# Who loads the second image's queries: 24 small loads moved from ScalarE's queue to SyncE's, and one pair of transposes moved later on VectorE

## The chip, the cores and the metric

The kernel runs on one core of a Trainium2 chip. The metric is the device time of one execution in microseconds (us). An execution has five instruction streams: TensorE (PE, with its weight loads shown as PEld), VectorE (DVE), ScalarE (ACT), GpSimd (POOL) and SyncE (SP). SP, ACT and POOL also issue DMA transfers; a DMA issued by SP or ACT stands in the profile as an instruction of the queue SPq or ACTq. The streams meet only through semaphores, and each executes its own instructions in the order in which they are written.

## The reference, cut to what is computed

```python
# attention in chunks of 64 tokens; q, k, v: (8, 8, 576, 64)
scores = scale * q_c @ k_c.T                  # 64 x 64 in each chunk of each head
attn = exp(scores - rowmax); attn = attn / (rowsum + 1e-9)
x = attn @ v_c                                # put together as (8, 576, 512)
# first layer: token mixing, then channel mixing
u = x + (relu(x.T @ w_tok1) @ w_tok2).T       # 576 -> 256 -> 576 tokens
x = u + relu(u @ w_ch1) @ w_ch2               # 512 -> 1536 -> 512 channels
# second layer: a gated layer
h = relu(x @ w_in); u, v = halves of h
v_n = (v - mean(v)) / sqrt(var(v) + 1e-6)
out = (u * (w_spatial @ v_n + b_spatial)) @ w_out
```

Everything is float32. A product is made of three passes over operands split in a high and a low part, so each weight matrix needs a high copy (written by ACT) and a low remainder (computed by POOL) before TensorE uses it.

## The kernel before, in words

There are eight images (b = 0 to 7) of 576 tokens. Attention works on five token tiles of an image, t = 0 to 4: four of 128 tokens and one of 64. "Tile (1, 2)" is tile 2 of image 1.

**The blocks.** After a prologue that does the attention and the token mixing of image 0, the channel mixing runs in nine blocks j = 0 to 8 of 512 tokens. A block is a list of 24 groups, `GROUPS`, in an order written out by hand: g = 0 up 0, g = 1 up 1, g = 2 down 0, g = 3 up 2, g = 4 down 1, g = 5 up 3 and so on, so that down 3 is g = 8, up 5 is g = 9, down 4 is g = 10 and up 9 is g = 17. "up f" computes a slice of the hidden layer (L1194), "down f" adds its product to the result (L1209); each is 12 matmuls. Behind each group TensorE does small side jobs of the next image's attention. For block 0 they stand in `PLAN_0` (L67): scores SC.0 behind g = 4, transposes of the probabilities PT.0 behind g = 6, values PV.0 and SC.1 behind g = 7, PT.1 behind g = 9, PV.1 and SC.2 behind g = 10, PT.2 behind g = 12, PV.2 and SC.3 behind g = 13, PT.3 behind g = 15, PV.3 and SC.4 behind g = 16, PT.4 behind g = 18.

**A tile's way.** The keys and queries of images 1 to 7 come in as blocks of 32 x 32 (tiles `kn`, `qn`, two buffers each), 16 DMAs for the keys and 16 for the queries of a tile: quarters z = 0 to 3 times head pairs g = 0 to 3. VectorE's `turn(b, t)` (L839) waits for all 16 of each and transposes the blocks, k_t first and then q_t, each into its only buffer. Then come the scores on TensorE, `softmax_shift` on VectorE (L849), the exponentials on ACT (L691), and `softmax_norm` on VectorE (L863): a sum (L868), a small addition (L870), a reciprocal (L872) and a product (L874). Only then can TensorE do PT. PT.t also waits until VectorE has taken PV.(t-1) out of its bank (L878, tile xl). On VectorE the order is written out: behind the scores of tile t come `softmax_shift(t)`, `turn(t + 1)`, `softmax_norm(t)`, the remainder xl of PV.(t-1), and then the remainder of the next hidden slice (L881, tile hidl).

**Who issues the loads.** SP issues all of a tile's 16 key DMAs and quarter 0 of its queries (4 DMAs); ACT issues quarters 1 to 3 (12 DMAs), three behind each of four successive groups. Only of tile (1, 0) does SP issue all 32. In block 0, `QUERIES[True]` (L726) lists the group at which ACT begins for each of the `TILES` (L727): (1, 3) at g = 5, (1, 4) at g = 8, (2, 0) at g = 12, (2, 1) at g = 16, (2, 2) at g = 20, (1, 1) at g = 0, (1, 2) at g = 3. Before the first query DMA of a tile that stands second or later after tile (1, 0), both queues wait until the turn of the tile before last has been done (L475, L735); SP waits alike before the keys (L481).

**SP's order in the prologue.** SP issues the channel weights in six pairs (w_ch1 and w_ch2 slices, 512 KB each), with these loads between them: behind pair 1 the 32 loads of tile (1, 0), behind pair 2 the 16 key loads of (1, 1) and its 4 query loads, behind pair 3 the 16 key loads of (1, 2); behind the last pair the 4 query loads of (1, 2). Then it goes on with keys and queries of (1, 3), (1, 4), (2, 0), (2, 1) and (2, 2).

**Weights of the channel mixing.** ACT makes the high copies of pair f right behind the activation of hidden slice f (L708, called at L744), and POOL follows with the two remainders (L611).

Of the kernel before, what the change touches and what calls it, by code (L numbers as in the profile page):

```python
# [18 lines left out]
def jobs(b, text):  # L19
    return [(kind, b, int(t)) for kind, t in (x.split(".") for x in text.split())]  # L20


def build(nc, q, k, v, w_tok1, w_tok2, w_ch1, w_ch2, w_in, w_spatial, b_spatial, w_out, out, x2_dram):
# [22 lines left out]
    def rows(t):  # L46
        return P if t < KS else REM
# [24 lines left out]
    def behind(j, g):  # L72

        if j > B - 1:
            return []
        side = jobs(j, (REST if j > 0 else REST_0).get(g, ""))
        if j < B - 1:
            return side + jobs(j + 1, (PLAN if j > 0 else PLAN_0).get(g, ""))
        return side + jobs(0, SPATIAL.get(g, ""))

    def scores_first(side):
        return [job for job in side if job[0] == "SC"] + [job for job in side if job[0] != "SC"]
# [46 lines left out]
    with ExitStack() as ctx:  # L129
# [10 lines left out]
        def place(name, shape, dt, at):  # L140
            t = nc.alloc_sbuf_tensor_at(name, shape, dt, offset=at)
            nbytes = 4
            for n in shape[1:]:
                nbytes *= n
            return t, at + (nbytes + 31) // 32 * 32
# [21 lines left out]
        qn, at = place("qn", [P, 2, PAIRS * P], F32, zone_a)  # L167
# [109 lines left out]
        def sem(name):  # L277
            return ctx.enter_context(nc.semaphore(name))
# [4 lines left out]
        q_loaded = [sem(f"q_loaded{t}") for t in range(NT)]  # L283
# [88 lines left out]
        q_in, k_in, v_in = q, k, v  # L372

        def later(b, t):

            return (b - 1) * NT + t
# [25 lines left out]
        def blocks(buf, b, t):  # L402
            return buf[:, later(b, t) % 2, 0:PAIRS * rows(t)]

        def block_of(buf, src, b, t, z, g):

            dst = blocks(buf, b, t)[z * BLK:(z + 1) * BLK, :].rearrange("p (g j e) -> p g j e", g=PAIRS, e=BLK)
            part = src[b, 2 * g + z // 2, t * P:t * P + rows(t), z % 2 * BLK:(z % 2 + 1) * BLK]
            return dst[:, g, :, :], part.rearrange("(j r) e -> r j e", r=BLK)
# [52 lines left out]
        def _(sp):  # L462
# [4 lines left out]
            def load_blocks(buf, src, b, t, loaded, quarters=range(4)):  # L467
                for z in quarters:
                    for g in range(PAIRS):
                        sp.dma_start(*block_of(buf, src, b, t, z, g)).then_inc(loaded[t], DMA)  # L470

            def load_q(b, t):
                if later(b, t) >= 2:

                    sp.wait_ge(q_t_ready, NT + later(b, t) - 1)  # L475

                load_blocks(qn, q_in, b, t, q_loaded, range(4) if (b, t) == (1, 0) else range(1))

            def load_k(b, t):
                if later(b, t) >= 2:  # L480
                    sp.wait_ge(k_t_ready, NT + later(b, t) - 1)  # L481
                load_blocks(kn, k_in, b, t, k_loaded)
# [13 lines left out]
            for g in range(NCW):  # L496
                cols = slice(g * CW_GROUP * P, (g + 1) * CW_GROUP * P)
                sp.dma_start(w1l_raw[:, :, cols],
                             w_ch1[:, cols].rearrange("(c p) n -> p c n", p=P)).then_inc(ch_loaded[2 * g], DMA)
                sp.dma_start(w2l_raw[:, g * CW_GROUP:(g + 1) * CW_GROUP, :],  # L500
                             w_ch2[cols, :].rearrange("(f p) n -> p f n", p=P)
                             ).then_inc(ch_loaded[2 * g + 1], DMA)
                if g == 1:
                    load_q(1, 0)
                    load_k(1, 0)
                if g == 2:
                    load_k(1, 1)
                    load_q(1, 1)
                if g == 3:
                    load_k(1, 2)  # L510
            load_q(1, 2)

            def store_x2(j):
# [8 lines left out]
            for j in range(B - 1):  # L522
                b = j + 1
# [123 lines left out]
        def _(act):  # L647
# [75 lines left out]

            QUERIES = {False: (2, 7, 11, 15, 19), True: (5, 8, 12, 16, 20, 0, 3)}  # L726
            TILES = ((1, 3), (1, 4), (2, 0), (2, 1), (2, 2), (1, 1), (1, 2))  # L727

            def load_queries(j, step, t, g):
                b = j + step  # L730
                if b >= B:
                    return
                if g == 0 and later(b, t) >= 2:

                    act.wait_ge(q_t_ready, NT + later(b, t) - 1)  # L735
                for z in range(1, 4):
                    nc.scalar.dma_start(*block_of(qn, q_in, b, t, z, g)).then_inc(q_loaded[t], DMA)

            for j in range(NB):
                for g, (kind, f) in enumerate(GROUPS):  # L740
# [4 lines left out]
                    for job in scores_first(behind(j, g)):  # L745
                        if job[0] == "SC":
                            exponentials(job[1], job[2])
                        else:
                            side_job(job)
                    for g0, (step, t) in zip(QUERIES[j == 0], TILES):  # L750
                        if g0 <= g < g0 + PAIRS:
# [86 lines left out]
        def _(dve):  # L838
            def turn(b, t):  # L839

                before = (b, t - 1) if t > 0 else (b - 1, KS)
                dve.wait_ge(side_full, number[("SC",) + before])
                for buf, dst, loaded, ready in ((kn, k_t, k_loaded, k_t_ready), (qn, q_t, q_loaded, q_t_ready)):
                    dve.wait_ge(loaded[t], b * (4 * PAIRS * DMA))
                    nc.vector.transpose(dst[:, :, 0:rows(t)].bitcast(U32),
                                        blocks(buf, b, t).bitcast(U32).rearrange("p (g s) -> p g s", g=PAIRS)
                                        ).then_inc(ready, 1)
# [15 lines left out]
            def softmax_norm(b, t):  # L863
                n, count = rows(t), tile_no(b, t) + 1
                dve.wait_ge(exp_done, count)
                p = prob_tile(b, t).rearrange("p g e k -> p (g e) k")
                sums, inverses = ssum[0:n, t % 2, :], srec[0:n, t % 2, :]
                nc.vector.reduce_sum(sums, p, AX_X).then_inc(sum_done, 1)  # L868
                dve.wait_ge(sum_done, count)
                nc.vector.tensor_scalar(sums, sums, 1e-9, None, ALU.add).then_inc(sum_eps, 1)  # L870
                dve.wait_ge(sum_eps, count)
                nc.vector.reciprocal(inverses, sums).then_inc(rec_done, 1)  # L872
                dve.wait_ge(rec_done, count)
                nc.vector.tensor_tensor(p, p, inverses.unsqueeze(2).to_broadcast([n, H, CHUNK]),  # L874
                                        ALU.mult).then_inc(prob_ready, 1)
# [4 lines left out]
            def low_relu(lo, src, hi):  # L880
                return nc.vector.scalar_tensor_tensor(lo, src, 0.0, hi.bitcast(F32), op0=ALU.max, op1=ALU.subtract)  # L881
# [29 lines left out]
            def hidden(j, f):  # L911
                n = j * KF + f
                dve.wait_ge(hid_hi, n + 1)
                low_relu(hidl[:, n % 2, :], hid[:, n % 2, :], hidh[:, n % 2, :]).then_inc(hid_lo, 1)

            def residual(j):

                for c in range(KC):
                    if c < KC - 1:
                        dve.wait_ge(acc_full, (KC - 1) * j + c + 1)  # L920
                    else:
                        dve.wait_ge(hid_used, KF * (j + 1))
                    nc.vector.tensor_tensor(x2[j % 2][:, c, :], acc[:, c, :], uh[j % 2][:, c, :].bitcast(F32),  # L923
                                            ALU.add).then_inc(acc_free, 1)
# [14 lines left out]
            for j in range(NB):  # L939
                if j > 0:  # L940
                    residual(j - 1)
                for g, (kind, f) in enumerate(GROUPS):
                    for job in scores_first(behind(j, g - 1) if g > 0 else []):
                        if job[0] == "SC":
                            softmax_norm(job[1], job[2])
                        elif job[0] == "PV":
                            side_job(job)
                    if j == 0 and g == 0:
                        turn(1, 0)
                    if kind == "up":  # L950
                        hidden(j, f)
                    for job in behind(j, g):
                        if job[0] == "SC":
                            softmax_shift(job[1], job[2])
                            n = later(job[1], job[2]) + 1
                            if n < (B - 1) * NT:
                                turn(1 + n // NT, n % NT)
                        elif job[0] in TWO_PART and job[0] != "PV":
                            side_job(job)
# [365 lines left out]
```

## Time and profile before

| | |
|---|---|
| median of 3 runs | 1254.31 us (1252.53 to 1255.63) |
| the profiled execution | 1254.31 us, its span 1252.5 us |
| granted clock of TensorE, mean | 1.0 |
| busy share of the span | PE 99%, PEld 85%, DVE 42%, ACT 27%, POOL 15% |

The span is the time between the first and the last instruction in the trace; the device time holds a little more. "Busy" of PE counts pipelined matmuls by modelled ends. The chain of waits is followed back from the last instruction. In the timelines a row merges neighbouring instructions of one line: first the start, then the time from the first start to the last end, and behind the count, in brackets, the idle time of the engine before it and what released it.

### The profile page before, as it was taken

Reading aid. Unit: us, or ns where it says so; the run is one execution under the profiler, and the core shown is the slowest. Engines: PE = TensorE matmul, PEld = TensorE weight load, DVE = VectorE, ACT = ScalarE, POOL = GpSimd, SP = SyncE. Lnnn points to the kernel's source line nnn. Section 1 sums busy time; section 2 is a strip of 40 time slices with the busy share of each in tenths; the row PEclk is TensorE's granted clock in tenths of the full one; section 3 lists DMA queues with packets and bytes.
Section 4 is the critical chain, followed back from the end, with each engine's and each line's share of the span. In section 5 each row is a group of like instructions: output and inputs, shape, how many; then the busy total and the mean of one; then the engine's idle time right before and its main releaser. Section 6 shows DMA issues by size and latency. Waiting matters only on the chain.

```text
span 1252.5 us, 20722 instructions
## 1 busy us (share of the span) xinstructions
PE 1235.2 (99%) x8385; PEld 1060.0 (85%) x8385; DVE 522.5 (42%) x1079; ACT 332.7 (27%) x647; POOL 190.0 (15%) x217
## 2 busy tenths in 40 slices
PE   6999999999999999999999999999999999999998
PEld 5878888888888888888888888889988998998997
DVE  5354344453353353453352222154633552562551
ACT  4442122121122121121121121124332442432322
POOL 4571111111111111111110141021000000000000
PEclk9999999999999999999999999999999999999999
DMA  9563123123222222232210231030210211111001
GB/s 227 120 125 61 49 45 58 49 49 54 52 48 50 52 52 47 52 55 44 53 31 1 72 115 34 1 110 1 77 72 5 77 42 34 45 66 42 1 9 68
DMA packets 191167, 70.34 MB, mean 56 GB/s; under 512 B 165664, under 2 KB 175520, under 8 KB 191072
## 3 DMA queue, kind: packets, MB, share of 16 engines
q1 hardware_dynamic: 133088, 53.55, 16.6%
q10 hardware_dynamic: 53376, 6.02, 3.4%
q0 software_dynamic: 4608, 9.45, 3.1%
q8 instruction: 66, 1.08, 0.4%
q14 instruction: 29, 0.24, 0.1%
HBM read 50.05 MB, written 18.87 MB: 55 GB/s over the span
## 4 chain that ended last, share of the span: by engine, by line
PE 97%; DMA 1%; DVE 1%; SPq 0%; ACT 0%; POOL 0%; ACTq 0%; issue 0%
PE acc L1220 24%; PE hid L1205 24%; PE acc L1078 15%; PE hid L1078 9%; PE side L1078 9%; PE side L1087 3%; PE side L1120 2%; PE side L1106 2%; PE side L1164 2%; PE side L1148 1%; PE side L1113 1%; PE side L1153 1%; DMA k_pro<-in_k 1%; PE hid L1087 1%; PE side L1116 0%; DMA qn<-in_q 0%
## 5 line engine op out<-in xcount | busy, mean ns | idle before, releaser
L881 DVE SCALAR_TENSOR_TENSOR hidl<-hid,hidh 128x512 fp32r<-128x512 f32 x108 | 74.5, 690 | 256.9 <-ACT hidh L698 256.9
L1220 PE MATMUL acc<-hidh,w2h 128*128 128x512 f32 x432 | 173.7, 402 | 0.0
L1220 PE MATMUL acc<-hidh,w2l 128*128 128x512 f32 x432 | 168.9, 391 | 0.0
L1220 PE MATMUL acc<-hidl,w2h 128*128 128x512 f32 x432 | 168.5, 390 | 0.0
L698 ACT ACTIVATE hidh<-hid 128x512 fp32r<-128x512 f32 x108 | 64.6, 598 | 295.9 <-PE hid L1205 289.2
L595 POOL DMA_DIRECT2D vn<-in_v x126 | 76.8, 617 | 331.3 <-PE side L1164 311.5
L1220 PEld LDWEIGHTS acc<-hidh,w2l 128*128 128x128 f32 x432 | 81.1, 188 | 17.8
L1205 PE MATMUL hid<-uh_a,w1h 128*128 128x512 f32 x240 | 95.8, 399 | 0.0
L1220 PEld LDWEIGHTS acc<-hidh,w2h 128*128 128x128 f32 x432 | 81.1, 188 | 16.8
L1220 PEld LDWEIGHTS acc<-hidl,w2h 128*128 128x128 f32 x432 | 81.2, 188 | 15.2
L1205 PE MATMUL hid<-uh_a,w1l 128*128 128x512 f32 x240 | 93.7, 391 | 0.0
L1205 PE MATMUL hid<-ul_a,w1h 128*128 128x512 f32 x240 | 93.6, 390 | 0.0
L1205 PE MATMUL hid<-uh_b,w1h 128*128 128x512 f32 x192 | 76.8, 400 | 0.0
L1205 PE MATMUL hid<-uh_b,w1l 128*128 128x512 f32 x192 | 75.0, 391 | 0.0
L1205 PE MATMUL hid<-ul_b,w1h 128*128 128x512 f32 x192 | 74.8, 390 | 0.0
L973 DVE BATCH_NORM_STATS2 bn<-nl_raw 128x6 f32<-128x512 f32 x32 | 22.2, 693 | 86.8 <-ACT nl_raw L769 86.8
L800 ACT CAST gh<-gl_raw 128x256 fp32r<-128x256 f32 x96 | 30.7, 352 | 97.0 <-DVE gl_raw L1028 97.0
L691 ACT ACTIVATE prob<-prob 128x512 f32<-128x512 f32 (+1 forms) x40 | 25.3, 633 | 108.4 <-DVE prob L859 108.4
L1205 PEld LDWEIGHTS hid<-uh_a,w1l 128*128 128x128 f32 x240 | 45.1, 188 | 9.7
L1205 PEld LDWEIGHTS hid<-uh_a,w1h 128*128 128x128 f32 x240 | 45.1, 188 | 9.5
L1205 PEld LDWEIGHTS hid<-ul_a,w1h 128*128 128x128 f32 x240 | 45.1, 188 | 8.8
L621 POOL TENSOR_TENSOR x_a<-x_a,ul_a 128x512 f32<-128x512 f32 x20 | 26.1, 1340 | 165.1 <-DVE x_a L923 165.1
(292 smaller groups left out, 2715.9 us busy)
## 6 DMA issues: line engine op xcount, KB each, us to landing
x2l_raw<-x_scratch SPq DMA_DIRECT2D x32, 256.0 KB, 5.0
out<-out_tile SPq DMA_DIRECT2D x32, 256.0 KB, 2.0
vn<-in_v POOLq DMA_DIRECT2D x126, 64.0 KB, 2.5
kn<-in_k SPq DMA_DIRECT2D x448, 16.0 KB, 1.9
qn<-in_q ACTq DMA_DIRECT2D x324, 16.0 KB, 2.0
w1l_raw<-in_moe_w_ch SPq DMA_DIRECT2D x6, 512.0 KB, 5.5
w2l_raw<-in_moe_w_ch SPq DMA_DIRECT2D x6, 512.0 KB, 7.0
x_scratch<-x_a SPq DMA_DIRECT2D x2, 1024.0 KB, 4.8
```

Source lines behind the costliest of these rows:

```text
L595: nc.gpsimd.dma_start(*v_part(b, t, h2, a)).then_inc(loaded[t], DMA)
L621: nc.gpsimd.tensor_tensor(x2[j % 2][:, c, :], x2[j % 2][:, c, :], ul[j % 2][:, c, :].bitcast(F32), ALU.add).then_inc(x2_ready, 1)
L691: nc.scalar.activation(p, p, ACT.Exp, scale=SCALE).then_inc(exp_done, 1)
L698: nc.scalar.activation(hidh[:, n % 2, :], hid[:, n % 2, :], ACT.Relu).then_inc(hid_hi, 1)
L800: a = nc.scalar.copy(gh[:, m % KC, to], gl_raw[:, m % KC, to])
L881: return nc.vector.scalar_tensor_tensor(lo, src, 0.0, hi.bitcast(F32), op0=ALU.max, op1=ALU.subtract)
L1078: last = nc.tensor.matmul(dst, w, x, start=(n == 0), stop=(n == len(operands) - 1))
L1087: nc.tensor.matmul(bank, w, x, start=(s == 0 and e == 0), stop=False)
L1106: nc.tensor.matmul(dst, w, x, start=(e == 0 and not turned_before), stop=False)
L1120: last = nc.tensor.matmul(dst, w, x, start=False, stop=(e == 2))
L1205: last = nc.tensor.matmul(hid[:, n % 2, :], w, x, start=(c == 0 and e == 0), stop=(c == KC - 1 and e == 2))
L1220: last = nc.tensor.matmul(acc[:, c, :], w, x, start=(f == 0 and e == 0), stop=(f == KF - 1 and e == len(ops) - 1))
```

## The change

It has three parts. SP issues all 16 query loads of tiles (1, 1) and (1, 2), and ACT none of them. The key loads of (1, 2), which stood on SP between the fourth and the fifth pair of weights, stand behind the sixth. VectorE does `turn(1, 0)` behind the hidden slice of g = 3 and no longer ahead of that of g = 0. With this ACT's list for block 0 is renumbered: (1, 3) still begins at g = 5, (1, 4) at g = 9 and no longer at 8, (2, 0) at g = 13 and no longer at 12; (2, 1) and (2, 2) stay.

```diff
-                load_blocks(qn, q_in, b, t, q_loaded, range(4) if (b, t) == (1, 0) else range(1))
+                load_blocks(qn, q_in, b, t, q_loaded, range(4) if b == 1 and t < 3 else range(1))
...
                 if g == 2:
                     load_k(1, 1)
                     load_q(1, 1)
-                if g == 3:
-                    load_k(1, 2)
+            load_k(1, 2)
             load_q(1, 2)
...
-            QUERIES = {False: (2, 7, 11, 15, 19), True: (5, 8, 12, 16, 20, 0, 3)}
-            TILES = ((1, 3), (1, 4), (2, 0), (2, 1), (2, 2), (1, 1), (1, 2))
+            QUERIES = {False: (2, 7, 11, 15, 19), True: (5, 9, 13, 16, 20)}
+            TILES = ((1, 3), (1, 4), (2, 0), (2, 1), (2, 2))
...
-                if g == 0 and later(b, t) >= 2:
+                if g == 0:
                     act.wait_ge(q_t_ready, NT + later(b, t) - 1)
...
-                    if j == 0 and g == 0:
-                        turn(1, 0)
                     if kind == "up":
                         hidden(j, f)
+                    if j == 0 and g == 3:
+                        turn(1, 0)
```

## Rows read from the trace of the kernel before

**Rows 1.** The page, busy time by engine.

```profile
PE 1235.2 (99%) x8385; PEld 1060.0 (85%) x8385; DVE 522.5 (42%) x1079; ACT 332.7 (27%) x647; POOL 190.0 (15%) x217
```

**Rows 2.** PE's waits over the whole run: total us, times, longest.

```profile
PE side L1153 <- DVE xl L878: 2.6, 1, 2.6
```

**Rows 3.** Windows by stage: busy time of each engine, granted clock, DMA share.

```profile
125.00:700.00 575.00, 575.00 (x4388) 477.70 (x4387) 240.24 (x436) 120.80 (x230) 96.25 (x128) 1.00 0.24 48
```

**Rows 4.** The chain of waits, 60 to 110 us: start, us, what.

```profile
63.37 0.62 PE side L1148 x32
...
72.43 5.05 DMA qn<-in_q
77.51 0.71 DVE q_t L845
...
78.82 1.77 DVE ssum L870
...
81.55 0.61 DVE xl L878
```

**Rows 5.** Timeline of PE: PT.1 and PT.4.

```profile
82.20 0.66 PE L1153 MATMUL side<-ident,prob 128*128 128x128 f32 x4 [2.56 <-DVE xl L878]
...
112.23 0.46 PE L1153 MATMUL side<-ident,prob 64*128 64x64 f32 x4
```

**Rows 6.** Timeline of SP's queue.

```profile
49.31 2.89 SPq L470 DMA_DIRECT2D qn<-in_q  x4
...
53.26 8.67 SPq L470 DMA_DIRECT2D kn<-in_k  x16
61.98 0.43 SPq L498 DMA_DIRECT2D w1l_raw<-in_moe_w_ch  x1
...
66.34 9.17 SPq L470 DMA_DIRECT2D kn<-in_k  x16
...
77.49 7.49 SPq L470 DMA_DIRECT2D kn<-in_k  x16
85.03 2.51 SPq L470 DMA_DIRECT2D qn<-in_q  x4
```

**Rows 7.** Landing times of SP's loads, line 470, 85 to 87.6 us.

```profile
DMA to landing us min/median/max: 1.9/2.1/2.5
```

**Rows 8.** Landing times of ACT's loads, line 737, 45 to 120 us.

```profile
DMA to landing us min/median/max: 1.6/2.3/6.4
```

**Rows 9.** Timeline of DVE, 40 to 115 us.

```profile
61.32 0.69 DVE L881 SCALAR_TENSOR_TENSOR hidl<-hid,hidh 128x512 fp32r<-128x512 f32 x1 [3.01 <-ACT hidh L698]
...
88.72 0.67 DVE L845 STREAM_TRANSPOSE q_t<-qn 128x512 uint32<-128x512 uint32 x1
...
108.63 0.66 DVE L845 STREAM_TRANSPOSE q_t<-qn 128x512 uint32<-128x512 uint32 x1
...
110.32 0.68 DVE L874 TENSOR_TENSOR prob<-prob,srec 64x512 f32<-64x512 f32 x1
110.93 0.68 DVE L878 TENSOR_TENSOR xl<-side,xh 128x512 fp32r<-128x512 f32 x1
```

**Rows 10.** Timeline of ACT, 40 to 115 us.

```profile
74.20 0.60 ACT L698 ACTIVATE hidh<-hid 128x512 fp32r<-128x512 f32 x1 [3.47 <-issue]
...
81.30 0.60 ACT L698 ACTIVATE hidh<-hid 128x512 fp32r<-128x512 f32 x1 [3.31 <-issue]
...
109.03 0.64 ACTq L737 DMA_DIRECT2D qn<-in_q  x1
```

**Rows 11.** Timeline of POOL, 40 to 115 us.

```profile
78.17 2.38 POOL L611 TENSOR_TENSOR w2l<-w2l_raw,w2h 128x1024 fp32r<-128x1024 f32 x1
82.91 2.41 POOL L611 TENSOR_TENSOR w1l<-w1l_raw,w1h 128x1024 fp32r<-128x1024 f32 x1 [2.36 <-ACT w1h L708]
```

**Rows 12.** Timeline of POOL, 826 to 865 us.

```profile
832.08 5.94 POOL L621 TENSOR_TENSOR x_a<-x_a,ul_a 128x512 f32<-128x512 f32 x4 [60.47 <-DVE x_a L923]
```

**Rows 13.** Timeline of DVE, 826 to 865 us.

```profile
833.72 6.05 DVE L878 TENSOR_TENSOR x2l<-x2l_raw,x2h 128x512 fp32r<-128x512 f32 x5
```

## The prediction

> **What bounds the kernel now.** I read the page first: TensorE is busy 99% of the span [rows 1]. Then I read who makes it wait. Behind the prologue its list of waits has one entry, 2.6 us before a PT job [rows 2], and the windows show TensorE busy for all of 575.00 us from 125 to 700 us at a granted clock of 1.00 [rows 3]. So there is no slack later that would swallow a delay: what TensorE loses in block 0 it loses for good. The other way round, the most that a cure can return is the one wait, 2.56 us before PT.1 at 82.20 [rows 5], 0.20% of the time.
>
> The chain of waits says where that wait comes from [rows 4]. The last query load of tile (1, 2), issued by ACT at 72.43, lands 5.05 us later; then VectorE transposes q_t from 77.51, sums, and comes at 78.82 to the small addition L870, which takes 1.77 us; L874 follows, and xl, whose end releases PT.1. So the time that counts is T, when the last query of (1, 2) has landed, 77.5 now. Everything between T and PT.1 is VectorE's written order: `turn(1, 2)` stands ahead of `softmax_norm(1, 1)`, on which PT.1 waits.
>
> **The change, part by part.**
>
> *ACT loses 24 issues.* They delay its activations now: hidh at 74.20 stands behind 3.47 us, and hidh at 81.30 behind 3.31 us, of idle put down to issue [rows 10]. Without them both can begin when TensorE is done. For the second (up 5) that is 82.20 - 2.56 = 79.64 [rows 5], so it moves 1.6 us earlier, to about 79.66. By itself this is worth nothing to TensorE, which waits for neither.
>
> *VectorE's turn(1, 0)* goes to the end of the third hidl, 61.32 + 0.69 = 62.0 [rows 9]. Its two transposes of 0.7 us, the second begun 0.6 behind the first, make k_t ready at 62.6 and q_t at 63.2. In its old place it held back nothing, since TensorE waits nowhere there [rows 2]. In the new one TensorE wants q_t for the scores at 63.37 [rows 4], so it is in time by a hair: cost 0 to 0.2 us, I take 0.
>
> *SP* now issues 16 and not 4 query loads of (1, 1) from 49.31. The pace of SP is 40 issues, keys and queries of two tiles, from 66.34 to 85.03 + 2.51 = 87.54: 0.53 us each [rows 6], occasional long ones included. So the 16 end at 57.8, ahead even of the turn of (1, 0). The six weight issues at some 0.5 us [rows 6] end at 60.8. The weights of pair 3 leave 5 us later than now; ACT wants them only behind hidden slice 3, an up and a down after 61.32 [rows 9], so I cost this at nothing; that cover holds as long as they land within some 5 us of their issue.
>
> Next comes load_k(1, 2), and it waits for the k_t of turn(1, 0), now 62.6. Before, these 16 loads began at 53.26 [rows 6], because the turn stood ahead of the first hidl and was long done. From 62.6 SP has 16 key and 16 query loads: 32 x 0.53 = 16.8 us, end 79.4. The last is issued at 79.0 and lands 2.1 us later [rows 7]: **T = 81.1 and not 77.5**. Bounds: without a single long issue, at 7.49 us for 16 as from 77.49 [rows 6], 62.6 + 15.0 - 0.5 + 2.1 = 79.3; at the 9.17 us for 16 of the worst row [rows 6], 62.6 + 18.3 - 0.5 + 2.3 = 82.7.
>
> *From T to PT.1.* Undisturbed, tile (1, 4)'s rows give q_t at 108.63 to the end of xl at 111.61 [rows 9], 3.0 us, so PT.1 would run at T + 3.1 = 84.2, 2.0 later than now. But L870 is not undisturbed even before: it arrives at 78.82 while POOL computes w2l (78.17 to 80.55 [rows 11]), and its 1.77 us end as POOL's instruction ends. It takes its turn behind POOL. The same is seen for a subtraction with both inputs in SBUF: five on VectorE take 6.05 us [rows 13], which at the 0.6 us pitch of such an instruction would be about 3.1, while POOL runs four of its own, stretched to 5.94 [rows 12]. They alternate, each waiting out the other's.
>
> Now place these. POOL's next pair of remainders begins 82.91 - 81.30 = 1.61 us behind the start of hidh [rows 10, 11], so with hidh at 79.66 it begins at 81.27: w1l to 83.68, w2l to 86.1. L870 arrives at T + 1.3 = 82.4, in the middle of w1l, and waits to 83.68. Then POOL's w2l begins, and L874, which like those five has both inputs in SBUF and arrives at 84.1, waits for its end at 86.1 and ends at 86.7; xl ends at 87.3. **PT.1 at 87.35 and not 82.20: 5.15 us lost.** Which T does this take? L870 meets w1l for T between 79.9 and 82.3, most of the range. For T from 79.5 to 79.9 only L874 meets w1l: PT.1 at 84.9, 2.7 lost. For T below 79.5 nothing meets: T + 3.1, at most 0.4 lost. Above 82.3 the loss is some 5.6.
>
> The Trainium skill (SBUF — State Buffer, "Who interferes with whom") says that VectorE and GpSimd share a pair of SBUF ports under an exclusive lock, which VectorE needs for a tensor_scalar in a two-port mode and, against a GpSimd instruction that reads SBUF, for one with two SBUF inputs. By this rule both L870 and L874 wait, 5.15; without it the loss would be 2.0. The trace agrees, by the 1.77 us of L870 and the 6.05 us of the five [rows 4, 13].
>
> *Tile (2, 0)'s queries begin on ACT at g = 13.* The last three are then issued behind g = 16. But `turn(2, 0)` is also at g = 16 on VectorE, ahead of norm(1, 4). ACT comes to them when it has dispatched the exponentials of (1, 4), in the slots that now serve (2, 1), of which the third begins at 109.03 [rows 10]. Landing takes 1.6 at least and 2.3 in the median [rows 8]; I take 2.1: 111.1 to 111.2. VectorE wants them at 108.63 [rows 9], so q_t and all behind it are 2.6 us late. xl ends at 111.61 now and PT.4 runs at 112.23 [rows 5], a reserve of 0.6: **2.0 us lost**. Bounds: 1.5 (landing 1.6) to 3.5 (landing 3.6, a busier DMA).
>
> *Tile (1, 4) at g = 9* ends behind g = 12 and is turned at g = 13; no cost. *SP behind T* is 79.4 + 20 x 0.53 = 90.0 with (1, 3), landed at 91.6. VectorE turns it at 88.72 now [rows 9], at 93.9 after the loss: in time, and the next two tiles alike, since SP's 10.6 us for a tile hardly exceed TensorE's (108.63 - 88.72) / 2 = 10.0 [rows 9]. Cost 0; if PT.1 lost only 0.4, up to 1.5 would come back here.
>
> **Sum**: 0 + 5.15 + 0 + 2.0 = 7.15 us. The profiled execution took 1254.31 us with a span of 1252.5, and it is the median too: 1254.31 + 7.15 = 1261.5 us, 0.57% slower.
>
> **The rivals.**
> 1. *T as computed, but POOL's pair lies elsewhere or T is early*, so that one or no lock is met: PT.1 loses 0.4 to 2.7, with 2.0 for PT.4 it is 1256.7 to 1259.0. For it: 0.5 us of T or of hidh decide. Against: the long issues on SP, about one in 20, push T into the lock. Chance 0.23.
> 2. *The change does what relieving ACT suggests*: SP brings (1, 2) in time, T at 76.4 or below, and the 2.56 us go: 1251.8, or 1253.8 with PT.4's wait. It decides from 32 issues taking under 12.2 us, 0.38 each. Against: no row of SP has such a pace, and the wait for turn(1, 0) is in the code. Chance 0.07.
> 3. *PT.1 as forecast, PT.4 free*, if the last queries of (2, 0) were issued well before the exponentials finish: 1259.5. Against: ACT waits for the shift of (1, 4) first. Chance 0.12.
> 4. *SP stays behind*, so that (1, 3), (1, 4) or (2, 0) wait again: 1263.5 to 1265. SP's 10.6 us a tile speak for it, the 2.3 us of reserve against. Chance 0.06.
>
> The forecast itself, both losses, has 0.52, with its own range 1260 to 1263.5.
>
> **How the numbers follow.** 1261.5 is the forecast. The range 1255.5 to 1263.5 takes in the forecast and rivals 1 and 3, with about a microsecond for the scatter of runs, and leaves out rivals 2 and 4. 0.3% is 3.8 us, about what a measurement of this kernel can tell from no change. Slower by more: the forecast, rivals 3 and 4 and a quarter of rival 1, less a little for errors of the sum, 0.72. Within: the rest of rival 1 and most of rival 2, 0.25. Faster: the only wait to be won is worth 0.20%, 0.03.
>
> **What would show it.** PT.1's wait for VectorE grows from 2.56 to about 7.7 us. The chain there names a query load issued by SP and not ACT, and VectorE's q_t of (1, 2) begins at 81 or so. L870 and L874 of tile (1, 1) are long, 1.3 and 2.6 us. hidh of up 5 begins at 79.7, and the waits for issue on ACT are gone. A second wait of some 2 us stands before PT.4, with a load by ACT behind it. SP's key loads of (1, 2) begin at 62.6. From PT.4 on, all of TensorE's work is shifted by one constant. I am wrong if SP issues faster than 0.45 us, if POOL lets VectorE pass twice, or if TensorE's clock falls in the longer wait; in the wait of 2.56 us it did not.

## The result, and the profile after

The changed kernel takes 1265.01 us in the median (1264.96 to 1266.58, 4 runs), the kernel before on the same chip 1253.48 us (1252.53 to 1255.63). The ratio is 1.0091, with a 95% interval of 1.0079 to 1.0103: 11.5 us slower. The forecast was 7.15 us slower, 1261.5, in a range of 1255.5 to 1263.5. The direction and both places are right, and the size is not. The profiled execution, from which the rows below come, took 1264.30 us.

TensorE's list of waits, of the changed kernel (total us, times, longest):

```profile
PE side L1152 <- DVE xl L877: 10.0, 2, 7.5
```

One wait of 2.56 us [rows 2] has become two of together 10.0. They are before PT.1 and PT.4. The timeline of PE shows them, and what the first matmuls behind them look like (line numbers are one lower than in the kernel before, from L510 on):

```profile
86.31 1.12 PE L1152 MATMUL side<-ident,prob 128*128 128x128 f32 x4 [7.50 <-DVE xl L877]
87.08 0.78 PE L1219 MATMUL acc<-hidh,w2h 128*128 128x512 f32 x1
87.65 0.63 PE L1219 MATMUL acc<-hidl,w2h 128*128 128x512 f32 x1
88.08 0.63 PE L1219 MATMUL acc<-hidh,w2l 128*128 128x512 f32 x1
...
90.74 0.39 PE L1219 MATMUL acc<-hidh,w2h 128*128 128x512 f32 x1
90.97 0.39 PE L1219 MATMUL acc<-hidl,w2h 128*128 128x512 f32 x1
...
120.81 0.53 PE L1152 MATMUL side<-ident,prob 64*128 64x64 f32 x4 [2.52 <-DVE xl L877]
...
122.28 0.63 PE L1204 MATMUL hid<-uh_a,w1l 128*128 128x512 f32 x1
```

Behind the wait, matmuls of one shape begin 0.43 us apart (87.65 to 88.08), from 90.74 on 0.23 apart. The windows of PE give the reason (stretch, its length, busy us, then the granted clock):

```profile
82.00:83.00 1.00, 0.00 (x0) 1.00 0.21 33
83.00:84.00 1.00, 0.00 (x0) 0.75 0.23 36
84.00:85.00 1.00, 0.00 (x0) 0.50 0.24 37
...
89.00:90.00 1.00, 1.00 (x4) 0.50 0.33 54
90.00:91.00 1.00, 1.00 (x5) 0.83 0.04 3
91.00:92.00 1.00, 1.00 (x35) 1.00 0.09 13
...
120.00:121.00 1.00, 0.19 (x3) 1.00 0.21 34
121.00:122.00 1.00, 1.00 (x6) 0.53 0.22 34
122.00:123.00 1.00, 1.00 (x4) 0.50 0.39 61
```

The granted clock fell from 1.00 to 0.50, that is from 2.4 to 1.2 GHz, when TensorE had been idle for some 4.7 us of its wait (the 0.75 of 83 to 84 us is half of each level), and stayed there through the rest of it and for some 4 us of matmuls. It fell again just behind the end of the wait of 2.52 us. The wait of 2.56 us before the change had left it at 1.00.

The chain of waits of the changed kernel, around both places:

```profile
78.15 1.88 DMA qn<-in_q
80.04 0.71 DVE q_t L844
80.76 0.58 DVE ssum L867
81.36 1.49 DVE ssum L869
82.87 0.21 DVE srec L871
83.10 2.55 DVE prob L873
85.65 0.61 DVE xl L877
...
114.52 0.46 ACTq L736
115.00 2.71 DMA qn<-in_q
117.73 0.71 DVE q_t L844
```

It is the chain of [rows 4] with SP in ACT's place at its head, with L873 (L874 before) long as well as L869 (L870 before), and with a second piece whose head is a query load that ACT issued at 115.00. The timelines of SP and of POOL:

```profile
61.66 9.27 SPq L470 DMA_DIRECT2D kn<-in_k  x16
70.98 7.60 SPq L470 DMA_DIRECT2D qn<-in_q  x16
```

```profile
80.45 2.35 POOL L610 TENSOR_TENSOR w1l<-w1l_raw,w1h 128x1024 fp32r<-128x1024 f32 x1 [2.00 <-ACT w1h L707]
82.76 2.35 POOL L610 TENSOR_TENSOR w2l<-w2l_raw,w2h 128x1024 fp32r<-128x1024 f32 x1
```

L869 begins at 81.36 and ends with POOL's w1l, L873 begins at 83.10 and does its work when w2l ends at 85.1.

**The books.** Block 0 began 1.00 us earlier in this execution (its first matmul at 45.40, before at 46.40). From there on, all in us:

| | before | after | lost |
|---|---|---|---|
| wait before PT.1 | 2.56 | 7.50 | 4.94 |
| PT.1 to the start of PV.1 | 3.33 | 5.21 | 1.88 |
| wait before PT.4 | 0 | 2.52 | 2.52 |
| PT.4 to the start of PV.4 | 3.36 | 4.88 | 1.52 |

The expectations below put 1.68 for the last; the rows give 1.52. The sum is 10.86; the token mixing of the next image begins 10.10 + 1.00 = 11.10 us later than before, so 0.24 is in other places. Some 0.2 of it is the late turn of (1, 0): SC.0 begins at 62.49, 17.09 us behind the start of block 0, and before at 63.30, 16.90 behind it. The spans differ by 10.0 (1262.5 and 1252.5), which is 11.1 less the 1.00 of the start and 0.1 at the end.

### The profile page after: what moved, and what is told of

Read it like the earlier page. It is cut to its first block, busy times and chain, and to the rows that moved or that the text cites. A ratio compares the mean times of both kernels' runs of the same rounds, so it can differ in the third digit from the quotient of the medians.

```text
span 1262.5 us, 20722 instructions
## 1 busy us (share of the span) xinstructions
PE 1236.5 (98%) x8385; PEld 1060.5 (84%) x8385; DVE 523.9 (41%) x1079; ACT 332.8 (26%) x647; POOL 189.9 (15%) x217
## 4 chain that ended last, share of the span: by engine, by line
PE 95%; SPq 2%; DVE 1%; DMA 1%; ACT 0%; issue 0%; POOL 0%; ACTq 0%
PE acc L1219 23%; PE hid L1204 23%; PE acc L1077 15%; PE hid L1077 9%; PE side L1077 9%; PE side L1086 3%; PE side L1119 2%; PE side L1105 2%; PE side L1163 2%; PE side L1147 1%; PE side L1112 1%; PE side L1152 1%; SPq L470 1%; DMA k_pro<-in_k 1%; PE hid L1086 1%; PE side L1115 0%
## 5 line engine op out<-in xcount | busy, mean ns | idle before, releaser
L1219 PEld LDWEIGHTS acc<-hidh,w2l 128*128 128x128 f32 x432 | 81.4, 188 | 17.9
```

Source lines behind the costliest of these rows:

```text
L1219: last = nc.tensor.matmul(acc[:, c, :], w, x, start=(f == 0 and e == 0), stop=(f == KF - 1 and e == len(ops) - 1))
```

## The experiments

### Put back (2, 0)'s start

```diff
-            QUERIES = {False: ..., True: (5, 9, 13, 16, 20)}
+            QUERIES = {False: ..., True: (5, 9, 12, 16, 20)}
```

> The changed kernel with one number put back: the queries of tile (2, 0) begin on ScalarE at g = 12 again. If the second wait of 2.52 us comes from those loads being issued behind the exponentials of tile (1, 4), it goes, and with it the stretch of half clock behind it (1.68 us): the time is about 1265.0 - 4.2 = 1260.8 us. Rival: the wait before PT.4 is SyncE's lateness (its key and query loads of (2, 0)); then it stays and the time is 1265. A second rival is that the lower clock is owed to the first wait alone; then only 2.5 us go, 1262.5.

Measured: 1261.06 us (1260.88 to 1261.47), ratio 1.0060 [1.0045, 1.0075]. TensorE's only wait for VectorE behind the prologue is the one before PT.1:

```profile
PE side L1152 <- DVE xl L877: 7.9, 1, 7.9
```

and from 110 to 130 us it is busy without a gap at 1.00. So about 4.0 us of the 11.5 come from beginning that tile's queries one group later: the wait, and the low clock behind it (2.52 + 1.52 in the books). In this execution T was later, and L869 met w2l, not w1l; L873 then passed freely. PT.1's wait was nearly the same.

### Keep TensorE busy through the waits

```diff
                         down(j, f)
+                    if j == 0 and g in FILL:          # {9: 30, 18: 10}
+                        fill(FILL[g], f)
                     for job in behind(j, g):
...
+            def fill(count, f):
+                n = f - 1 if f % 2 == 1 else f
+                pe.wait_ge(hid_lo, n + 1)
+                for m in range(count):
+                    nc.tensor.matmul(hid[:, n % 2, :], w1h[:, m % KC, 0:P], uh[0][:, m % KC, :], start=True, stop=True)
```

> The changed kernel, with 30 idle matmuls ahead of PT.1 and 10 ahead of PT.4 that write a hidden bank which the next up overwrites; nothing else is changed. TensorE works through both waits. If what the sum of the prediction lacked is the granted clock (1.88 us behind the first wait, 1.68 behind the second), the clock stays at 1.00 and the time is about 1265.0 - 3.6 = 1261.5 us, the waits for VectorE shrinking to 0.7 us and 0.2. Rival: the slower matmuls behind the waits come from something else (DMA traffic, SBUF); then the time stays at 1265 and the matmuls behind PT.1 stay 0.43 us apart.

Measured: 1261.81 us (1261.02 to 1261.84), ratio 1.0064 [1.0048, 1.0079]. 40 matmuls more, and 3.2 us less. PE's timeline and its windows behind the first place:

```profile
79.28 6.96 PE L1231 MATMUL hid<-uh_a,w1h 128*128 128x512 f32 x30
87.49 0.66 PE L1152 MATMUL side<-ident,prob 128*128 128x128 f32 x4 [1.25 <-DVE xl L877]
```

```profile
87.00:88.00 1.00, 0.51 (x5) 1.00 0.64 141
88.00:89.00 1.00, 1.00 (x7) 1.00 0.56 120
```

PT.1 comes no earlier, but the clock is 1.00 behind it, and from PT.1 to PV.1 it is 3.34 us, as in the kernel before. The DMA traffic there, 120 to 141 GB/s, is like that of the changed kernel (110 to 156), so it did not make the matmuls slow; the clock did.

### The same ahead of PT.1 alone

The edit is the one before with `FILL = {9: 30}`.

> The changed kernel with the 30 idle matmuls ahead of PT.1 alone. It tells whether the low clock behind PT.4's wait of 2.5 us needs the long wait ahead of it. If it does, both stretches of half clock go and the time is that of the fill at both places, about 1261.5 us; if each wait stands for itself, only the first goes: 1265.0 - 1.9 = 1263.1 us.

Measured: 1263.30 us (1262.07 to 1264.73), ratio 1.0078 [1.0062, 1.0094], close to the forecast for waits that stand for themselves, but the interval holds the other forecast too. The executions differ: in the profiled one (1262.07) the clock did not fall behind PT.4, after a wait of 2.29 us,

```profile
120.13 0.46 PE L1152 MATMUL side<-ident,prob 64*128 64x64 f32 x4 [2.29 <-DVE xl L877]
```

```profile
120.00:121.00 1.00, 0.87 (x6) 1.00 0.23 36
```

with a mean clock of 1.000, while the other three (1262.39, 1264.20 and 1264.73) had 0.998, 0.997 and 0.998. So a wait of this length before PT.4 is not always followed by a fall. Whether the clock fell behind PT.4 in the other three is not shown: a mean does not say where it fell. In the profile of the fill at both places it is 0.997 too, with 1.00 all through block 0, and all of the fall lies in the prologue:

```profile
16.00:18.00 2.00, 1.30 (x33) 0.50 1.23 207
18.00:20.00 2.00, 1.98 (x16) 0.50 1.11 306
```

### Make POOL step aside

```diff
             for n, (hi, raw, lo) in enumerate(W_FIRST):
...
+                if n == WL_TOK + 10:
+                    pool.wait_ge(prob_ready, tile_no(1, 1) + 1)
                 pool.wait_ge(whi, n + 1)
```

> The changed kernel, with GpSimd waiting for the probabilities of tile (1, 1) before it computes the last pair of remainders. If VectorE's L869 and L873 are long because GpSimd holds the shared port, they fall from 1.47 and 2.55 us to 0.17 and 0.69 and PT.1's wait from 7.5 to 4.3 us; the time falls by 3.2 us plus what less low clock gives, up to 1.9: 1260 to 1262. Rival: they are long for another reason; then nothing changes, 1265.

Measured: 1262.52 us (1261.39 to 1264.77), ratio 1.0073 [1.0055, 1.0092]. DVE's and PE's timelines:

```profile
80.67 0.71 DVE L846 STREAM_TRANSPOSE q_t<-qn 128x512 uint32<-128x512 uint32 x1 [4.86 <-DMA qn<-in_q]
...
81.99 0.17 DVE L871 TENSOR_SCALAR ssum<-ssum 128x8 f32<-128x8 f32 x1
...
82.43 0.69 DVE L875 TENSOR_TENSOR prob<-prob,srec 128x512 f32<-128x512 f32 x1
```

```profile
83.78 1.11 PE L1154 MATMUL side<-ident,prob 128*128 128x128 f32 x4 [4.50 <-DVE xl L879]
```

1.47 and 2.55 us have become 0.17 and 0.69, T is within 0.2 us of its place behind the start of block 0, and PT.1's wait is 3.0 us shorter. The Trainium skill (SBUF — State Buffer, "Who interferes with whom") says that the later of two instructions that need the shared port waits for the whole of the other; these rows agree. The time fell by 2.5 us, less than the 3.2 hoped for. With four executions of each the two intervals overlap, so it is the rows that show the cause and not the time. The clock fell all the same (0.73 in the window from 82 to 83 us, 0.50 from there to 89): from PT.1 to PV.1 it took 5.88 us, and in the changed kernel 5.21. PT.4's wait was 2.97 us.

### Put back the turn of (1, 0)

```diff
+                    if j == 0 and g == 0:
+                        turn(1, 0)
                     if kind == "up":
                         hidden(j, f)
-                    if j == 0 and g == 3:
-                        turn(1, 0)
```

> The changed kernel with turn(1, 0) back ahead of the first hidden slice. SyncE then doesn't wait for it, begins the keys of (1, 2) at 60.2 and not at 61.66, and T is 78.6 and not 80.0. By my account that is just early enough for L869 and L873 to pass ahead of GpSimd's pair at 80.45: PT.1 at 81.7, its wait 3.0 and not 7.5 us, and little or no low clock there, 1265.0 - 4.5 - 1.9 = 1258.6 us. If L873 meets the pair all the same, PT.1 is at 84.1 and the time 1261 to 1263. Rival: the late turn costs nothing, because SyncE is late by its number of issues alone; then 1265.

Measured: 1265.80 us (1263.98 to 1266.57), ratio 1.0096 [1.0075, 1.0118]: my forecast of 1258.6 failed, and the time is that of the rival. SP's timeline:

```profile
61.09 9.18 SPq L470 DMA_DIRECT2D kn<-in_k  x16
70.32 8.64 SPq L470 DMA_DIRECT2D qn<-in_q  x16
```

In this execution SP had finished the weights only at 61.05; it began the keys 1.0 us earlier against the start of block 0, not 1.5. The 32 issues then took 17.9 us (61.09 to 78.96) and not 16.9, with long ones of up to 1.5 us among them, and T was 0.24 us earlier in all. L869 and L873 met POOL just the same, 1.55 and 2.55 us. So the wait that the prediction put ahead of these loads ("it waits for the k_t of turn(1, 0)") is real: in the changed kernel SP issued its last weights at 59.65 and the first key at 61.66. But in this execution its removal brought T only 0.24 us forward and PT.1's wait (7.49 us) not at all, because the issues behind it were slower. What an earlier start is worth when they are not was not measured.

### The renumbering of (2, 0) alone, in the kernel before

```diff
-            QUERIES = {False: ..., True: (5, 8, 12, 16, 20, 0, 3)}
+            QUERIES = {False: ..., True: (5, 8, 13, 16, 20, 0, 3)}
```

> The kernel before with one number of the change: the queries of tile (2, 0) begin on ScalarE at g = 13 and not 12. If this part alone makes the wait before PT.4, a wait of about 2.0 to 2.5 us appears there and nothing else moves: 1253.5 + 2.0 to 2.5 = 1255.5 to 1256, and 1257.5 if the clock falls behind it as it did in the changed kernel. Rival: 1253.5, if the wait needs the rest of the change.

Measured: 1259.72 us (1255.08 to 1261.36), ratio 1.0043 [1.0028, 1.0059]. PE's timeline, and its windows behind the second wait:

```profile
81.79 0.99 PE L1153 MATMUL side<-ident,prob 128*128 128x128 f32 x4 [3.06 <-DVE xl L878]
...
116.42 0.69 PE L1153 MATMUL side<-ident,prob 64*128 64x64 f32 x4 [2.93 <-DVE xl L878]
```

```profile
116.00:117.00 1.00, 0.58 (x4) 0.55 0.23 36
117.00:118.00 1.00, 1.00 (x4) 0.50 0.21 33
```

The wait before PT.4 appears with that one number. Its price is more than its length: the clock stayed at 0.50 for some 6 us behind it, and PT.4 to PV.4 took 6.04 us and not 3.36, 2.7 more. It fell behind PT.1 too, where PT.1 to PV.1 took 4.93 and not 3.33. So the 7 us of this execution are not the price of the second wait alone. One execution in six had a mean clock of 1.000, and that one took 1255.08, near the forecast without any low clock; the other five, at 0.994 to 0.998, took 1258.67 to 1261.36. Where the clock fell in those that have no profile is not known.

The code up to PT.1 is that of the kernel before, so the clock can fall behind PT.1 there as well, though it did not in its profile. This fits the runs of the kernel before on this chip: six of 25 took 1255.25 to 1259.16 us, all with a mean clock below 1.000, and the median is 1252.79. But many of the faster ones have a mean below 1.000 too, and none of these six has a profile, so it is not shown.

### Versions meant to be faster

Against the changed kernel, the first gives ACT its 12 loads of (1, 2) back, but early, and puts the turn and the key loads where they were:

```diff
-                load_blocks(..., range(4) if b == 1 and t < 3 else range(1))
+                load_blocks(..., range(4) if b == 1 and t < 2 else range(1))
...
+                if g == 3:
+                    load_k(1, 2)
-            load_k(1, 2)
             load_q(1, 2)
...
-            QUERIES: True: (5, 9, 13, 16, 20)      TILES: ..., (2, 2)
+            QUERIES: True: (5, 9, 12, 16, 20, 1)   TILES: ..., (2, 2), (1, 2)
...
+                    if j == 0 and g == 0:
+                        turn(1, 0)
...
-                    if j == 0 and g == 3:
-                        turn(1, 0)
```

> A version meant to beat both. SyncE issues all queries of (1, 1), ScalarE keeps its 12 of (1, 2) but issues them from g = 1, turn(1, 0) and the keys of (1, 2) stand where they stood before, (1, 4) begins at g = 9, (2, 0) at g = 12. T falls to about 74, so q_t of (1, 2) no longer waits. But L870 and L874 of tile (1, 1) then come at 76 to 77 and meet GpSimd's fourth pair (73.7 to 78.5): PT.1 waits about 1.2 us and not 2.56. Time 1253.5 - 1.4 = 1252.1 us. If relieving ScalarE were all that counts and there were no port, 1250.9.

> The version before it, and GpSimd waits for the probabilities of tile (1, 1) before the second remainder of its fourth pair. By the port theory PT.1 then waits for nothing or next to it: 1253.5 - 2.56 = 1250.9 us, 1.2 below the version without it. Rival: no difference between the two.

The second version is the first with POOL's wait, whose edit is shown at the end of this section.

Measured: 1252.92 us, ratio 0.9996 [0.9987, 1.0005], and with POOL's wait 1252.90 us, 0.9995 [0.9984, 1.0007]. No measurable gain, though in the profile of the first PT.1 waited only 1.29 us. The chain of waits of the second says why its own wait was still 2.29 us, with low clock behind it (its row of PE is shown first):

```profile
81.53 1.11 PE L1155 MATMUL side<-ident,prob 128*128 128x128 f32 x4 [2.29 <-DVE xl L880]
```

```profile
71.26 7.15 DMA qn<-in_q
78.43 0.71 DVE q_t L847
```

T was not 74. The last of SP's own four query loads landed 7.15 us after its issue, behind the 2 MB of weights issued just ahead of the four. The Trainium skill (DMA: Bandwidth & Descriptors, "Issuing engines are not separate DMA queues") puts the loads of all queues on the same 16 engines. The trace agrees: ACT's four query loads issued from 67.6 to 70.6 us, on another queue, took up to 7.2 us.

```profile
DMA to landing us min/median/max: 3.4/5.8/7.2
```

So in the next version SP's four go ahead of the last pair:

```diff
                 if g == 3:
                     load_k(1, 2)
+                if g == 4:
+                    load_q(1, 2)
-            load_q(1, 2)
```

> The shared version with SyncE's four query loads of (1, 2) issued ahead of the last pair of weights instead of behind it. In the shared versions these four landed 6.1 and 7.1 us after their issue behind 2 MB of weights; behind 1 MB they land in about 4.5, T is about 74 and q_t waits for nothing. L870 still meets GpSimd's fourth pair: PT.1 waits 1.2 us or less, 1252.8 - 1.4 = 1251.4 us.

> The same, and GpSimd waits as well. Both causes of the one wait are gone: PT.1 waits 0 to 0.3 us, the clock stays at 1.00 and the time is 1252.8 - 2.5 = 1250.3 us. Rival: the waits only move to PT.2, because GpSimd's remainders and value loads come later; then 1252.

Measured: 1252.30 us, ratio 0.9991 [0.9983, 1.0000], and with POOL's wait **1251.43 us** (1250.78 to 1252.06), ratio **0.9983 [0.9974, 0.9991]**, against 1253.16 of the kernel before. DVE's timeline in the two, without POOL's wait and with it:

```profile
77.30 1.95 DVE L871 TENSOR_SCALAR ssum<-ssum 128x8 f32<-128x8 f32 x1
```

```profile
77.68 0.17 DVE L873 TENSOR_SCALAR ssum<-ssum 128x8 f32<-128x8 f32 x1
```

In the first, q_t no longer waits (the loads of 16 KB that SP issued from 66 to 72.5 us landed in at most 5.2 us), and PT.1 still waits 1.31 us, with the addition held up beside POOL. In the second TensorE waits for VectorE nowhere in block 0; by ratio it gains 2.1 us (1.1 to 3.3) of the 2.56 that there were to gain. The slowest of its twelve executions took 1252.06, while five of the 29 of the kernel before took 1255.14 to 1257.96.

POOL's wait in the kernel before, by itself:

```diff
+                if n == WL_TOK + 9:
+                    pool.wait_ge(prob_ready, tile_no(1, 1) + 1)
                 pool.wait_ge(whi, n + 1)
```

> The kernel before, and GpSimd waits for the probabilities of tile (1, 1) before the second remainder of its fourth pair; nothing else. If L870's 1.77 us are the port, it takes 0.17, PT.1's wait falls from 2.56 to about 1.0 us, and the time by 1.6 us, to about 1251.2 where the kernel before has 1252.8. Rival: the wait stays at 2.56.

Measured: 1253.13 us, ratio 0.9995 [0.9986, 1.0003]. In its profile the addition takes 0.17 us and PT.1's wait is 1.23 us, so the cause is gone:

```profile
79.39 0.17 DVE L872 TENSOR_SCALAR ssum<-ssum 128x8 f32<-128x8 f32 x1
```

```profile
81.18 0.66 PE L1155 MATMUL side<-ident,prob 128*128 128x128 f32 x4 [1.23 <-DVE xl L880]
```

but the time is not measurably lower. A gain of 1.3 us lies within the interval, and 2.56 is the wait of one execution of the kernel before; how long it usually is was not measured. The forecasts of all five of these versions were too low, by 0.8 to 2.0 us.

## Why the prediction was right in direction and wrong in size

**T.** Forecast 81.1, or 34.7 us behind the start of block 0 at 46.40; measured 80.04, which is 34.6 behind 45.40. The pace of 0.53 us held: 32 issues in 16.9 us, forecast 16.8. In other executions of the same queue order T was up to 2.7 us later (the fill at both places), with long issues and late landings. So the mechanism is right, and that it came out to 0.1 us is luck.

**From T to PT.1.** Forecast 5.15 us lost, measured 4.94. The meeting with POOL's pair was foretold to 0.2 us a piece (L869 1.47 and not 1.3, L873 2.55 and not 2.6), and stepping POOL aside took it away. That L874 would wait as well came from [rows 12, 13] and not from any row of a softmax; it was the larger part (2.55 us).

**Tile (2, 0).** Forecast 2.0 us, measured 2.52; the landing was 2.7 us and not 2.1. That the renumbering makes this wait is shown by its removal and by making it alone.

**SyncE behind T, the weights, tile (1, 4).** Costed at nothing; no wait appeared there. The late turn of (1, 0): forecast 0 in a range to 0.2, and SC.0 was 0.19 us late.

**The step that failed** is the sum, "0 + 5.15 + 0 + 2.0": it lacks a term. I had written of TensorE's clock that it did not fall in the wait of 2.56 us, and put its falling in the longer one among the things that would make me wrong, with no price and no rival. It fell behind both waits and cost 1.88 + 1.52 = 3.4 us; keeping TensorE busy gave 3.2 back. With it the sum is 7.46 + 3.4 = 10.9, against 11.5 in the medians. Of the remaining 0.6, 0.24 is in other places of block 0, and 0.4 is less than the scatter of the runs: the kernel before had medians of 1253.48 and, in later comparisons, 1252.8 and 1253.2, and the forecast stood on one execution of 1254.31. The price could have been estimated from the pitch of the matmuls in the kernel before: at half clock twelve of 0.23 us take another 2.8 at each wait. That would have set the upper end above 1265. The profiles gave 1.4 to 2.7 us at each of ten falls, up to the next PV.

**The rivals.** None came. Of the second, relieving ACT did free its activations (hidh at 78.85 follows TensorE with no issue in between, 1.45 us earlier against the start of block 0), and POOL's pair came forward by the same amount, into VectorE's way.

**Open:** what makes the clock fall behind one wait and not behind another. Of the waits before PT.1 and PT.4 in the thirteen profiles, the five of 0.8 to 1.3 us left it at 1.00 and the seven of 2.93 us and more were all followed by a fall. In between both happened: it held at 2.56 (before) and 2.29 (fill ahead of PT.1), and fell at 2.29 (shared version with POOL's wait), 2.33 (turn put back) and 2.52 (changed). The falls came 2.0 to 4.9 us after TensorE had gone idle. The length of the wait alone does not decide.

## What to carry to other kernels

A load that is moved from one issuing queue to another brings with it all its issue slots: here 0.53 us each, 16.9 us for one tile's keys and queries, and then every load behind it. Before moving an issue one group later, look at the group in which its data is consumed, and on which side of an activation the issuing engine reaches it; one number cost 4 us here. And price a new wait of TensorE as its length plus, as the upper end, the matmuls behind it at half clock: here 1.4 to 2.7 us, behind ten of the twelve waits of 2.29 us and more, and nothing behind the five of up to 1.3 us.

## What the runs showed of the hardware that was not expected

- A wait of TensorE of 2.3 to 2.6 us is followed by half clock in some profiles and not in others (2.29 us did both). Idle matmuls in place of a wait kept the clock at 1.00.
- VectorE's addition on 128x8 elements took 1.2 to 2.05 us when it came while GpSimd subtracted, and 0.17 otherwise; a product on 128x512 behind it took 2.55 and not 0.69.
- The last of four query loads of 16 KB took 6.1 and 7.15 us to land behind 2 MB of weights, and loads on another queue in that stretch up to 7.2; in a quiet stretch it was 1.9 to 2.1.
